# Four vector instructions of the second early tile, moved to other places of the plan's chain

## The reference

```python
def reference(...):
    # 1. linear attention with decay, 4 x 8 heads, 768 positions, head size 48
    for t in range(S):
        y[:, :, t] = r_t @ (state + (u * k_t) v_t);  state = w * state + k_t v_t
    # 2. dense layer on 3072 tokens: h = max(x@w1, x@w2, x@w3); x = h @ w_out   (384 -> 768 -> 384)
    # 3. top-2 of 8 experts (384 -> 1024 -> 384)
    noisy = x @ w_gate + log1p(exp(x @ w_noise)) * noise
    top2, weights = the two largest of noisy, softmax of the two
    for e in range(8), k in range(2):
        out[mask] += weight[mask, k] * (max(x[mask] @ w1[e], 0) @ w2[e])
```

## Time and profile before

| | |
|---|---|
| three runs | 885.52, 887.44, 887.62 us (median 887.44) |
| the profiled execution | 880.52 us, of which the span of the trace 878.4 us |
| PE busy | 864.7 us, 98% |
| DVE busy | 451.2 us, 51% |
| ACT, POOL busy | 271.8 us, 391.6 us |
| granted TensorE clock | 1.00 |
| second early tile's first product | 444.91 to 453.54 us of the span |

### The profile page before, as it was taken

The page is one execution under the profiler, slowest core; times in us unless marked ns, Lnnn a source line. Parts: engine busy times, 40 slices in busy tenths (PEclk is TensorE's granted clock), DMA queues, the critical chain, the costliest instruction groups (busy, mean ns, idle before and its releaser), DMA issues. The chain is left out here.

```text
span 878.4 us, 19557 instructions
## 1 busy us (share of the span) xinstructions
PE 864.7 (98%) x6540; PEld 842.4 (96%) x6541; DVE 451.2 (51%) x1100; ACT 271.8 (31%) x522; POOL 391.6 (45%) x380
## 2 busy tenths in 40 slices
PE   7999999999999999999999999999999999999997
PEld 5899999999999999999999999999999999999997
DVE  8773656546465655637574564352535335264322
ACT  4532323223231322225414342431414233143211
POOL 5344425343342544234454555453544526365543
PEclk9999999999999999999999999999999999999999
DMA  8795112221221221032115622624326252442222
GB/s 208 191 306 147 40 37 66 63 67 51 62 53 47 66 55 38 1 135 56 46 47 190 196 61 56 185 59 145 115 57 186 79 190 74 126 150 62 73 63 68
DMA packets 103765, 86.08 MB, mean 98 GB/s; under 512 B 60634, under 2 KB 93090, under 8 KB 103696
## 3 DMA queue, kind: packets, MB, share of 16 engines
q1 hardware_dynamic: 83152, 31.75, 15.1%
q0 software_dynamic: 12416, 26.28, 9.7%
q10 hardware_dynamic: 8128, 27.13, 9.4%
HBM read 70.46 MB, written 21.35 MB: 105 GB/s over the span
## 5 line engine op out<-in xcount | busy, mean ns | idle before, releaser
L1445 PE MATMUL ps<-yh,wh 128*128 128x384 f32 x432 | 147.5, 342 | 2.0 <-ACT x_sb L1225 2.0
L1336 ACT ACTIVATE gh<-ps 128x384 fp32r<-128x384 f32 x136 | 66.9, 492 | 264.6 <-PE ps L1447 264.6
L1445 PE MATMUL ps<-xgh,w1h 128*128 128x384 f32 (+1 forms) x456 | 145.0, 318 | 0.0
L1447 PE MATMUL ps<-xgh,w1l 128*128 128x384 f32 (+1 forms) x456 | 145.0, 318 | 0.0
L1446 PE MATMUL ps<-xgl,w1h 128*128 128x384 f32 (+1 forms) x456 | 144.9, 318 | 0.0
L1447 PE MATMUL ps<-yh,wl 128*128 128x384 f32 x432 | 144.5, 335 | 0.0
L1446 PE MATMUL ps<-yl,wh 128*128 128x384 f32 x432 | 144.4, 334 | 0.0
L1085 DVE SCALAR_TENSOR_TENSOR gl<-ps,gh 128x384 fp32r<-128x384 f32 x136 | 75.8, 557 | 126.7 <-ACT gh L1336 126.7
L1445 PE MATMUL ps<-w2h,gh 128*128 128x384 f32 x408 | 138.3, 339 | 0.9 <-DVE gl L1079 0.9
L1446 PE MATMUL ps<-w2l,gh 128*128 128x384 f32 x408 | 136.5, 335 | 0.0
L1447 PE MATMUL ps<-w2h,gl 128*128 128x384 f32 x408 | 136.5, 335 | 0.0
(11 more groups left out here) (205 smaller groups left out, 1511.9 us busy)
## 6 DMA issues: line engine op xcount, KB each, us to landing
ew_raw<-ew ACTq DMA_DIRECT2D x28, 768.0 KB, 4.6
v_sb<-vN SPq DMA_DIRECT2D x24, 192.0 KB, 2.6
out<-zrow SPq DMA_DIRECT2D x1, 4608.0 KB, 15.5
x_rows<-x_sb ACTq DMA_DIRECT2D x8, 576.0 KB, 3.9
kn_sb<-kN SPq DMA_DIRECT2D x20, 192.0 KB, 3.2
k_raw<-kT SPq DMA_DIRECT2D x48, 72.0 KB, 1.9
wraw<-moe_w SPq DMA_DIRECT2D x6, 576.0 KB, 8.6
r_raw<-rT SPq DMA_DIRECT2D x44, 72.0 KB, 2.1
```

The source lines that it names most:

```text
L1336: act.activation(gh[:, f, :], ps[f % 4][:, 0:T], ACT.Relu).then_inc(gh_ok, 1)
L1445: pe.matmul(o, ah, bh, start=start, stop=False)
L1447: return pe.matmul(o, al, bh, start=False, stop=stop)
```

## The change

The three low parts that stood behind `make_plan()` move into it, and the one that stood in it moves further ahead. Nothing is added or taken away.

```diff
                 for n, row in ((0, before), (1, tiles), (2, first), (3, full)):
                     own(dve.tensor_copy(plan_f[:, n, 0:NE], row))
+                early_low(1, 0)
                 own.settle()
                 t, inside, at, third, over = (spread[:, n] for n in range(5))
...
                 own(dve.scalar_tensor_tensor(third, at, float(ET), third, ALU.add, ALU.add))
+                early_low(1, 1)
                 own.settle()
                 own(dve.tensor_tensor(at, at, inside, ALU.mult))
                 own(dve.tensor_tensor(third, third, inside, ALU.mult))
                 own.settle()
-                early_low(1, 0)
+                early_low(1, 2)
                 for n, row in enumerate((at, third)):
                     own(dve.tensor_reduce(tile_f[:, n, :], row.rearrange("p e m -> p m e"), AX.X, ALU.add))
+                early_low(1, 3)
                 own.settle()
                 own(dve.tensor_copy(tile_at[:, :, :], tile_f[:, :, :]))
                 own.settle()
...
             make_plan()
-            for q in range(1, 4):
-                early_low(1, q)
             dve.wait_ge(rows_out, 32)
             early_row(1, 0)
```

## The result

| comparison | before | after | ratio, 95% interval |
|---|---|---|---|
| the first (8 and 8 runs) | 887.55 us (885.19 to 889.95) | 891.5 us (891.02 to 892.78) | 1.0046 [1.0033, 1.0058] |

Forecast was 886.9 us in a range of 884.3 to 889.0, and no change. It came out 0.46% slower and outside the range.

What follows compares the result with a forecast made beforehand. PE, busy 864.7 of 878.4 us, was taken to bound the kernel by its instruction order. Removing a 1.16 us stall, less the gathers' wait and restart, saves 0.5: 887.44 - 0.5 = 886.9 us, range 884.3 to 889.0.

Steps and rivals of the forecast that it cites:

- What bounds the kernel, and what the stall costs: PE's instruction order is the critical path from 455 us; its stall on a low part costs 1.16 us.
- The replay of DVE: Second early tile's low parts on DVE start at 448.02, 452.52, 453.89 and about 455.49 us, removing PE's stall.
- What is late next: PE waits for gathers before the first planned tile's transposes until about 459.95 us, leaving 0.51 of 1.16 us saved.
- the first bullet of the replay: Low part 0, behind four casts on DVE, starts at 448.02 us, its high part ready at 447.92; plan 0.69 us later.
- it does not do what it says: Low part 0 makes DVE wait for ACT, delaying plan and later low parts; 887.4 us, part of the 0.17 chance.
- The step from the profiled execution to the median: The same 0.5 us taken from the profiled 880.52 us was subtracted from the runs' median, 887.44 us, giving 886.9.
- The slower rival: Moved low parts beside POOL's gather issues lengthen all three to 2.15 us; 890.2 us, chance 0.05.

Runs made afterwards that it cites:

- late_after: Kernel after the edit plus nine spare copies on ACT, making the second early tile's first high part about 6 us late; 885.58 us, ratio 1.0062 to before.
- before_fourth: The kernel before, unchanged, timed and traced again in the third later group, which had hold-ups; 891.75 us, ratio 1.0003.
- low0_late: Kernel after the edit with low part 0 put back directly ahead of low part 1; 878.92 us, ratio 0.9988; repeated with hold-ups 890.75 us, 0.9996.

## Why the prediction was wrong

- **What bounds the kernel, and what the stall costs.** Right. From the transposes to the end it is 417.8 to 418.0 us in every trace. The stall was worth 1.29 us in P2 where I had 1.16 and a possible 0.07.
- **The replay of DVE.** Right to 0.03 us in each of the four starts, while ACT is on time.
- **What is late next.** Right in kind: the wait on the gathers took part of the gain, 0.29 us by the engine's row and 0.45 us in P2, where I had 0.65. SP's load, which waits for the same signal, starts at 459.1 there, as PE's transposes do; the reading of the earlier trace rows as the landing time holds. The gain is 0.84 us in the stretch (15.65 to 14.81) and 0.9 us and 0.4 us in the medians of the two clean groups; I had 0.5.
- **The failed step is the first bullet of the replay:** "With a hand-over of 0.06 to 0.23 it starts between 447.98 and 448.15". I took the time of the high part from the one trace and bounded only the hand-over. By its own figures DVE arrives 0.04 us before its operand, so the wait had no margin; but what is queued behind it (twelve plan steps, three low parts, and PE behind these) was not priced for an operand that is late, only for one on time. The rival "it does not do what it says" named this very wait and gave it the time of no change, 887.4 us. With a high part 6 us late the replay itself would have given low part 1 at 448.0 + 6 + 4.5 = 458.5, and a PE that is on time some 4 us of waiting for pair 1: a time above the range. In its place the runs showed, in the trace after, DVE 5.39 us idle in front of low part 0, low part 1 4.9 us behind it, and PE waiting 2.07 us for pair 1; with a late high part by construction (late_after) the loss is 5.7 us, against 1.1 in the order before.
- **The step from the profiled execution to the median.** I subtracted 0.5 from both, and passed over that the three runs lay 5.0 to 7.1 us above the trace. A trace that is quicker than every timed run shows a condition that the runs do not have. Those 5 to 7 us were probably hold-ups, as before_fourth has them; it isn't shown for the first comparison, whose only trace of before is the clean one.
- **The slower rival,** POOL's gathers lengthened by DVE, did not happen: in every trace each of the three issues took 1.00 to 1.25 us, where the rival had 2.15.

What stays open: why PE is held up; why in some groups only; and how the 4.0 us of the first comparison divide. P2 of the trace after is 3.19 us over the least, of which 2.31 are waits for low parts; it is 1.90 us longer than in the trace before, a small part of the 11.9 between the two traces. But the hold-ups before and in P1 differ between executions, the kernel before may have had fewer of them there (887.55 us against 890.85 and 891.75), and the later comparisons with hold-ups gave only 1.6 and 2.2 us.

## What to carry to other kernels

Before moving an instruction that waits to the front of a chain, ask what the chain did while the operand was under way: independent steps ahead of a wait are its cover, and the same steps behind it are its price. Put it where its operand has been ready for some time and the consumer still has some; here low part 0 had 5.5 us between the two, and low0_late puts it in the last third of them. When the timed runs and the trace differ by more than the effect in question, find out what the difference is before reading margins of a tenth of a microsecond from the trace.

## What the runs showed of the hardware

In two of the four later groups all runs of every kernel took longer; the kernel before took 891 and 892 us where the other two had 880. In each of their traces ACT waited 14.5 to 15.0 us in front of its first work on the second early tile, where 9.6 is normal, and 8.8 to 8.9 us in front of an `x_sb` copy; in that tile's first product PE paused two to four times by 0.2 to 1.05 us with nothing to wait for. The places are the same in each kernel, so they seem to hang on the program; whether they appear differed between the groups, and as each group had one chip, the chip and the moment are not told apart. The granted clock takes its share: the mean over all runs of the kernel before is 0.995 in the two groups with hold-ups and 0.9995 in the others, which makes at most some 4 of the 11 to 12 us (an estimate, 0.0045 of 890 us; PE stood idle for part of the time at the lower clock). And a wait of some 3 us on PE costs more than itself: in late_after the clock was at 1.00 until 456.5 and at the 1.2 GHz level from 457.0 to 463.5, 5 us of it behind the end of the wait at 458.43.
